# Folding the last query tile of an attention item by halves of its keys, in a kernel that runs attention beside two feed-forward layers

## The reference

```python
scores = scale * np.matmul(q, k.transpose(0, 1, 3, 2))
mask = (pos[:, None] // 64) >= (pos[None, :] // 64)
scores = np.where(mask, scores, -1000000000.0)
scores = scores - np.max(scores, axis=-1, keepdims=True)
attn = np.exp(scores)
attn = attn / (np.sum(attn, axis=-1, keepdims=True) + 1e-09)
x = np.matmul(attn, v)                      # to [2304 tokens, 512]
h = x @ moe_w_in                            # 512 x 2048
g = np.where(h >= 1, h, np.where(h <= -1, 0.0, (h + 1) ** 2 / 4.0))
x = g @ moe_w_out                           # 2048 x 512
h = x @ moe2_w_in
out = (h * np.cos(h)) @ moe2_w_out
```

## Time and profile before

| | |
|---|---|
| median of three runs | 1042.07 us |
| profiled execution, its own time | 1043.83 us |
| span of that execution, first to last instruction | 1041.7 us |
| PE busy | 997.8 us, 96% of the span |
| DVE busy | 657.9 us, 63% |
| ACT busy | 590.0 us, 57% |
| POOL busy | 422.7 us, 41% |
| mean granted TensorE clock | 0.988 of full |

### The profile page before, as it was taken

How to read it: one execution, slowest core, us unless ns; L and a number is a source line. 1 busy time by engine, 2 the same in 40 slices (tenths; PEclk the granted TensorE clock), 3 DMA queues, 4 the chain that set the end, 5 groups by cost and what they waited for, 6 DMA issues and landing times.

```text
span 1041.7 us, 19484 instructions
## 1 busy us (share of the span) xinstructions
PE 997.8 (96%) x7360; PEld 941.2 (90%) x7360; DVE 657.9 (63%) x1422; ACT 590.0 (57%) x1232; POOL 422.7 (41%) x446
## 2 busy tenths in 40 slices
PE   5699999999999999999999999999999999999997
PEld 4588999899999999999999999899999999999995
DVE  5668777766766767667642369665565656656553
ACT  5578766666666666666642357545445454545542
POOL 4558755655555554654632222222221222222221
PEclk9889999999999999999999999999999999999999
DMA  5235321221211212211110045010110101001000
GB/s 166 92 109 171 98 76 59 70 73 49 89 53 49 93 49 67 75 58 64 69 48 22 21 157 187 1 41 0 40 24 16 40 0 40 12 29 40 0 21 21
DMA packets 30885, 62.27 MB, mean 60 GB/s; under 512 B 3680, under 2 KB 11872, under 8 KB 30816
## 3 DMA queue, kind: packets, MB, share of 16 engines
q1 hardware_dynamic: 29664, 57.16, 17.2%
q10 hardware_dynamic: 1152, 4.19, 1.1%
HBM read 51.90 MB, written 9.44 MB: 59 GB/s over the span
## 4 chain that ended last, share of the span: by engine, by line
PE 79%; DVE 9%; ACT 5%; issue 3%; DMA 1%; POOL 1%; ACTq 0%; POOLq 0%; DVEq 0%
PE hidden L1155 33%; PE acc L1174 18%; PE acc L1188 13%; PE heads_out L1078 4%; PE scores L1032 3%; PE turned L1046 3%; PE scores L1033 2%; DVE neg_max L827 1%; PE heads_out L1046 1%; DVE wout_lo L892 1%; ACT probs L643 1%; DVE q_parts L816 1%; DVE x_lo L906 1%; PE hidden L1122 1%; DVE win_lo L885 1%
## 5 line engine op out<-in xcount | busy, mean ns | idle before, releaser
L568 POOL TENSOR_TENSOR g_lo<-work,g_hi 128x512 fp32r<-128x512 f32 x144 | 186.9, 1298 | 431.5 <-ACT g_hi L740 431.5
L1155 PE MATMUL hidden<-x_hi,win_hi 128*128 128x256 f32 x1136 | 321.9, 283 | 1.1 <-DVE work L917 1.1
L1155 PE MATMUL hidden<-x_hi,win_lo 128*128 128x256 f32 x1136 | 316.8, 279 | 3.8 <-DVE q_parts L816 2.8
L1155 PE MATMUL hidden<-x_lo,win_hi 128*128 128x256 f32 x1136 | 316.3, 278 | 0.0
L1155 PEld LDWEIGHTS hidden<-x_hi,win_hi 128*128 128x128 f32 x1136 | 214.6, 189 | 5.3 <-DVE work L917 1.3
L1155 PEld LDWEIGHTS hidden<-x_hi,win_lo 128*128 128x128 f32 x1136 | 214.6, 189 | 4.6 <-DVE q_parts L816 3.3
L1155 PEld LDWEIGHTS hidden<-x_lo,win_hi 128*128 128x128 f32 x1136 | 214.9, 189 | 3.8
L1188 PE MATMUL acc<-g_hi,wout_hi 128*128 128x256 f32 x576 | 167.5, 291 | 0.2 <-ACT y_stage L723 0.2
L1188 PE MATMUL acc<-g_hi,wout_lo 128*128 128x256 f32 x576 | 161.3, 280 | 3.0 <-DVE pt_lo L844 3.0
L538 POOL TENSOR_SCALAR probs<-probs,row_inv 64x576 f32<-64x576 f32 (+2 forms) x160 | 105.1, 661 | 136.8 <-DVE row_inv L839 135.9
L1188 PE MATMUL acc<-g_lo,wout_hi 128*128 128x256 f32 x576 | 160.5, 279 | 0.0
(11 more groups left out here) (99 smaller groups left out, 1841.2 us busy)
## 6 DMA issues: line engine op xcount, KB each, us to landing
qk_raw<-qk_late SPq DMA_DIRECT2D x32, 448.0 KB, 3.3
qk_raw<-qk_early SPq DMA_DIRECT2D x32, 256.0 KB, 2.6
v_raw<-v_late SPq DMA_DIRECT2D x32, 160.0 KB, 3.3
x_raw<-x_scratch SPq DMA_DIRECT2D x9, 512.0 KB, 3.4
out<-y_stage SPq DMA_DIRECT2D x36, 128.0 KB, 2.4
x_raw<-w_in SPq DMA_DIRECT2D x8, 512.0 KB, 3.6
y_stage<-w_out SPq DMA_DIRECT2D x8, 512.0 KB, 3.5
x_scratch<-y_stage ACTq DMA_DIRECT2D x8, 512.0 KB, 2.7
```

Of the source, the lines that this page charges most:

```text
L568: nc.gpsimd.tensor_tensor(g_lo[:, m % G_RING, :], work[:, m % 2, :], g_hi[:, m % G_RING, :], ALU.subtract).then_inc(g_lo_made, 1)
L1155: last = nc.tensor.matmul(into, w[:, p, c, half * P:(half + 1) * P], x[:, c, :], start=(i == 0), stop=(i == len(products) - 1))
```

## The change

Three parts, and a table of orders that goes with them.

**The fold.** Tile 4 of a late item becomes 128 rows by 320 keys. The keys are laid out in DRAM in the order of chunks 4, 0, 2, 1, 3. Rows 0 to 63 hold the 64 queries against chunks 4, 0 and 2, and rows 64 to 127 the same queries against nothing (the first 64 columns, masked), 1 and 3. PE gets this by two products into the same bank, with the queries shifted by 64 columns among zeros (`q_folded`): 320 columns and then 256. The row maxima and the row sums of the two halves are exchanged by copies of one column between the halves of the partitions (`max_swap`, `sum_swap`). Three transposes of 128 by 128 turn it, where five of 64 rows did. The queries of a late item are 384 columns where they were 320, with zeros among them. The score banks of late items alternate, so the first tile's scores no longer wait for the last exponential of the item before.

**Two buffers.** `k_hi`, `k_lo`, `qk_raw` and `v_raw` hold two late items. The raw data of the first two late items are loaded together after the split of item 31, and after that two items ahead. Keys of a late item are split at slots -14 and -13, before at -10 and -11.

**The last tile.** Pair 7 is made right behind pair 6, into a bank of `scores`; the last pair's 12 matmuls finish one accumulator bank and then the other, and each bank is copied and stored by itself.

```diff
-QKV_COLS = (2 * EARLY, LATE + S)
+LATE_Q = LATE + BLOCK
+QKV_COLS = (2 * EARLY, LATE_Q + S)
...
+KEY_ORDER = (4, 0, 2, 1, 3)
+KEY_COLS = [slice(P * j, min(S, P * (j + 1))) for j in KEY_ORDER]
+FOLD = LATE
...
-    return min(S, P * (i + 1))
+    return FOLD if i == 4 else P * (i + 1)
...
+def chunk_col(i, j):
+    return (0, 2 * P, P, 3 * P)[j] if i > 1 else P * j
...
-    "turn_c": (0, 0, 19), "weigh": (12, 18, 21), "k_hi": (-5, -9, -10), "q_hi": (-5, -8, -11),
...
-    "pt_lo_b": (0, 0, 18), "pt_lo_c": (0, 0, 19), "add": (13, 18, 23), "k_lo": (-4, -10, -11),
...
-    "begin": (16, -2, -6), "v_lo": (7, 7, 6),
...
+    "turn_c": (0, 0, 19), "weigh": (12, 17, 21), "k_hi": (-6, -9, -14), "q_hi": (-4, -8, -11),
...
+    "pt_lo_b": (0, 0, 18), "pt_lo_c": (0, 0, 19), "add": (13, 18, 23), "k_lo": (-4, -10, -13),
...
+    "begin": (16, -3, -10), "v_lo": (8, 8, 7),
...
+def keys_before(n):
+    return n - 3 if n < ALONE else -1 if n == ALONE else n - 2
...
-    if n + 1 < ITEMS:
-        yield n + 1, k - slots_of(n)
+    for m in range(n + 1, min(n + 3, ITEMS)):
+        yield m, k - sum(slots_of(i) for i in range(n, m))
...
-def slots_made(heads):
-    return {made_at(s, heads): s for s in range(PAIRS)}
+def slots_made(heads, last=False):
+    made = {made_at(s, heads): s for s in range(PAIRS)}
+    if last:
+        made[made_at(PAIRS - LAG - 2, heads) + 2] = made.pop(made_at(PAIRS - LAG - 1, heads))
+    return made
...
+        qk_raw = sb("qk_raw", [P, 2 * QKV_COLS[1]], F32)
+        v_raw = sb("v_raw", [P, 2 * 5 * D], F32)
+        q_parts = sb("q_parts", [P, 3, BLOCK + LATE_Q], F32R)
+        k_hi = sb("k_hi", [P, 2, S], F32R)
+        k_lo = sb("k_lo", [P, 2, S], F32R)
...
+        def hidden_of(m, last=False):
+            return scores[:, 0, :] if last and m == PAIRS - 1 else hidden[:, m % 2, :]
...
+        def q_tile(n, e):
+            at = 2 * BLOCK + BLOCK + P * e if late(n) else BLOCK + P * e
+            return q_parts[:, n % 3, at:at + P]
...
+        def q_folded(n, half):
+            at = BLOCK * (1 - half)
+            return q_parts[:, n % 3, at:at + P]
...
-            return (k_hi, g_hi[:, 0, EARLY:2 * EARLY], g_hi[:, 1, EARLY:2 * EARLY])[place_of(n)]
+            return (k_hi[:, n % 2 if n >= ALONE else 0, :], g_hi[:, 0, EARLY:2 * EARLY], g_hi[:, 1, EARLY:2 * EARLY])[place_of(n)]
...
+            return scores[:, (i + n) % 2 if late(n) else i % 2, 0:ext_of(i)]
...
+        def probs_fold(n, a):
+            at = probs_at(n, 4) + (BLOCK, BLOCK + P, 0)[a]
+            return probs[:, at:at + P]
...
+            def same_kind_of_raw(n):
+                return n < ITEMS and n not in (HEADS, HEADS + 1)
...
             def after_split(n):
                 sp.wait_ge(q_lo_made, n + 1)
                 sp.wait_ge(k_lo_made, n + 1)
-                if n + 2 < HEADS:
+                if same_kind_of_raw(n + 2):
                     load_qk(n + 2)
-                elif HEADS - 1 <= n < ITEMS - 1:
-                    load_qk(n + 1)
+                if n == HEADS - 1:
+                    load_qk(HEADS)
+                    load_qk(HEADS + 1)
...
             def store_out(t):
-                sp.wait_ge(acc_read, t + 2)
                 staged = y_stage[:, :].rearrange("p (a m) -> p a m", a=2)
                 for e in range(TOK // D):
+                    if e == 0 or (e == 2 and t == 2 * TILES - 1):
+                        sp.wait_ge(acc_read, t + 2 + e // 2)
                     row = out_rows(t - TILES, e)
                     sp.dma_start(out[row:row + D, :], staged[(e % 2) * D:(e % 2) * D + D, e // 2, :]).then_inc(y_stored, 16)
...
-                if user_before(n) >= 0:
-                    act.wait_ge(scores_made, first_tile(user_before(n) + 1))
+                if keys_before(n) >= 0:
+                    act.wait_ge(scores_made, first_tile(keys_before(n) + 1))
...
             def row_max(n, i):
                 tile = first_tile(n) + i - tiles_of(n)[0]
                 dve.wait_ge(scores_made, first_tile(n) + 2 if n < ALONE else tile + 1)
+                bank = bank_of(n, i)
+                if i == 4:
+                    hidden_part = bank[BLOCK:P, 0:BLOCK]
+                else:
+                    at = chunk_col(i, i) + BLOCK
+                    hidden_part = bank[0:BLOCK, at:at + BLOCK]
+                nc.vector.memset(hidden_part, MASKED).then_inc(masked, 1)
+                dve.wait_ge(masked, tile + 1)
+                col = stat(n, i)
+                top = neg_max[:, col:col + 1]
                 if i < 4:
...
+                    nc.vector.tensor_reduce(out=top, in_=bank, axis=AX_X, op=ALU.max, negate=True).then_inc(max_made, 1)
+                    return
+                m = n - HEADS + 1
+                nc.vector.tensor_reduce(out=top, in_=bank, axis=AX_X, op=ALU.max, negate=True).then_inc(half_max_made, 1)
+                dve.wait_ge(half_max_made, m)
+                for to, source in ((0, BLOCK), (BLOCK, 0)):
+                    nc.vector.tensor_copy(max_swap[to:to + BLOCK, :],
+                                          neg_max[source:source + BLOCK, col:col + 1]).then_inc(max_swapped, 1)
+                dve.wait_ge(max_swapped, 2 * m)
+                nc.vector.tensor_tensor(top, top, max_swap[:, :], ALU.min).then_inc(max_made, 1)
+            def inverse(n, i):
+                done = first_tile(n) + i - tiles_of(n)[0] + 1
                 dve.wait_ge(exp_made, done)
                 col = stat(n, i)
...
+                sums, inverses = row_sum[:, col:col + 1], row_inv[:, col:col + 1]
+                if i < 4:
+                    nc.vector.tensor_scalar_add(sums, sums, EPS).then_inc(sum_guarded, 1)
+                else:
+                    for to, source in ((0, BLOCK), (BLOCK, 0)):
+                        nc.vector.tensor_copy(sum_swap[to:to + BLOCK, :],
+                                              row_sum[source:source + BLOCK, col:col + 1]).then_inc(sum_swapped, 1)
+                    dve.wait_ge(sum_swapped, 2 * (n - HEADS + 1))
+                    nc.vector.scalar_tensor_tensor(out=sums, in0=sums, scalar=EPS, in1=sum_swap[:, :], op0=ALU.add,
+                                                   op1=ALU.add).then_inc(sum_guarded, 1)
                 dve.wait_ge(sum_guarded, done)
...
+                nc.vector.reciprocal(inverses, sums).then_inc(inv_made, 1)
...
+            def read_last(t, a, stored):
+                dve.wait_ge(acc_half_made, a + 1)
+                if a == 0:
+                    dve.wait_ge(y_stored, stored)
+                nc.vector.tensor_copy(y_stage[:, a * 512:(a + 1) * 512], acc[:, a, :]).then_inc(acc_read, 1)
...
-                        pe.wait_ge(exp_made, first_tile(n))
+                        pe.wait_ge(exp_made, first_tile(n) - (1 if n > ALONE else 0))
+                elif e == 1 and n > ALONE and not banks_seen(n):
+                    pe.wait_ge(exp_made, first_tile(n))
                 elif e == 2:
-                    pe.wait_ge(exp_made, first_tile(n) + 2)
+                    pe.wait_ge(exp_made, first_tile(n) + 1)
                 if i == 4:
...
+                    even, odd = q_folded(n, 0), q_folded(n, 1)
+                    width = S - FOLD
+                    products = [(bank, even, k[:, 0:FOLD]) for k in (k_hi_of(n), k_lo_of(n))]
+                    products += [(bank[:, FOLD - width:FOLD], odd, k[:, FOLD:S]) for k in (k_hi_of(n), k_lo_of(n))]
                 else:
...
+                    first = BLOCK if late(n) else 0
+                    products = [(bank, q_tile(n, e), k[:, first:first + ext_of(i)]) for k in (k_hi_of(n), k_lo_of(n))]
+                for which, (into, q, k) in enumerate(products):
+                    last = nc.tensor.matmul(into, q, k, start=(which == 0), stop=(which == len(products) - 1))
                 last.then_inc(scores_made, 1)
...
             def turn(n, e):
                 pe.wait_ge(probs_made, first_tile(n) + e + len(tiles))
...
+                if e == 2:
+                    sources = [probs_fold(n, a) for a in range(3)]
+                elif late(n):
+                    sources = [probs_chunk(n, tiles[0], j) for j in range(tiles[0] + 1)]
+                else:
+                    sources = [probs_chunk(n, i, j) for i, j in ((0, 0), (1, 0), (1, 1))]
+                for at, source in enumerate(sources):
+                    last = nc.tensor.transpose(turned_of(n, e)[:, at * P:(at + 1) * P], source, ident[:, :])
                 last.then_inc(turned_made, 1)
...
+            def use_last(t):
+                p, slot = PAIRS - 1, (PAIRS - 1) % G_RING
+                pe.wait_ge(g_lo_made, PAIRS * t + p + 1 + 2)
+                for a in range(TOK // P):
+                    for half in range(2):
+                        at = half * TOK + a * P
+                        for i, (w, g) in enumerate(((wout_hi, g_hi), (wout_hi, g_lo), (wout_lo, g_hi))):
+                            last = nc.tensor.matmul(acc[:, a, :], g[:, slot, at:at + P], w[:, p, half, :], start=False,
```

(19 more changed lines are left out.)

152 lines of the change are left out of this document (60 added, 92 removed).

## The result

The changed kernel takes 1074.84 us in the median of four runs (1074.04 to 1079.51) against 1042.43 us for the kernel before (1041.71 to 1043.18): a ratio of 1.032, 95% interval 1.0289 to 1.0351. It is 32 us slower; 12 us faster had been forecast.

The account below looks back on a forecast made before the run. PE's issue of matmuls was taken to bound the kernel. Fold -9.6, buffers -1.1, handover +1.1 and last tile -2.2 summed to -11.8 us, from the median of 1042.07 to 1030.3 us; range 1025 to 1037 us.

Parts of the forecast that it names:

- The fold on the other engines, at nothing: Late items: DVE gets about 0.65 us more per item, hidden beside PE's matmuls; ACT and POOL get less; cost nothing.
- The fold on PE: Tile 4 of late items: three transposes for five save 0.30 us in each of 32 items, 9.6 us.
- the rival by columns: Tile 4's transposes are paid by columns, so nothing is saved there; kernel lands at 1041.2 us; chance 6%.
- The four scores, cost "at nothing": Tile 4's four score products have 1152 columns in all before and after, so no change in time.
- Two buffers: Late items: PE's waits for the keys' low part go, as their split comes sooner; -1.1 us, ends -3.3 and 0.
- The handover: Start of late items: the wait for item 32's load is paid earlier, at a weighing; +1.1 us, ends 0 and +3.
- The last tile: End of program: less waiting for `g_lo` 1.0, shorter last copy 0.6, earlier stores 0.6; -2.2 us, ends -0.5 and -3.5.
- The table at 0 (±1.5): Early items' slots move by one or two on ACT, DVE and POOL; cost 0, with 1.5 us either side.
- The slower rival: New PE wait ahead of tile 4's transposes, low keys delaying POOL's normalising; at 0.6 us per item 1049.5 us; chance 8%.
- released by POOL: Sign that the forecast is wrong: PE idle ahead of tile 4's transposes, released by POOL, in many items.
- over 80%: Sign that the forecast is wrong: DVE busy for over 80% in the late stretch.

Follow-up runs that it names:

- no_swap: one_port_832 without the exchange of the two halves' maxima and sums, so the reference isn't computed for those 64 queries: 1029.90 us, ratio 0.9885.
- one_port_832: Changed kernel with the minimum and the sum taking the swapped column as a per-partition scalar, and 960 B of padding ahead of ident: 1041.32 us, ratio 0.9982.
- old_table: Changed kernel with the kernel before's table of slots put back: 1069.42 us, ratio 1.0262.
- tail_alone: Kernel before with only the last tile's part of the change: 1039.35 us, ratio 0.997.
- act_sums: one_port_832 with the two copies that exchange the halves' sums moved from DVE to ACT: 1052.94 us, ratio 1.0094.
- pad_64: Kernel before with 64 B of unused padding ahead of ident, no instruction changed: 1061.00 us, ratio 1.0177.
- all_64: Kernel before with 64 B of padding ahead of the weights, so that everything moves together: 1042.38 us, ratio 0.9999.

## Why the prediction was wrong

**The sum that failed.** Forecast 1030.3 us; measured in steps: place 16.2, the minimum behind POOL 17.3, the exchange 11.4 us. With them the forecast becomes 1075.2 us, and 1074.8 was measured. Without all three stands no_swap at 1029.9. That both agree within 0.4 us is partly luck: the terms that are left were off by up to some 2 us each and the table by 5.6 us, as shown below, and no_swap leaves out a step that the forecast had in it.

**"The fold on the other engines, at nothing"** is the step that failed worst, and in two places: priced at nothing, it cost 17.3 and 11.4 us. The minimum was priced at 147 ns from the row of an operation on one column. That row has one input; the minimum has two, and the table puts `k_lo` beside it. The trace of before had the pair of rows that shows it: of two instructions of one form in the second layer, both beside POOL's `g_lo` in 70 of 72 cases, the one with an input in PSUM takes 688 ns, and the one with both in SBUF takes 1166.

```profile
L929 DVE SCALAR_TENSOR_TENSOR work<-probs,work 128x512 f32<-128x512 f32 x72 | 84.0, 1166 | 2.5
...
L926 DVE SCALAR_TENSOR_TENSOR work<-probs,hidden 128x512 f32<-128x512 f32 x72 | 49.5, 688 | 7.5
```

The second place is the argument that 0.65 us per item "hides beside PE's matmuls" since DVE had 22 us idle in 75. The lengths were right: a copy takes 148 ns, the reduction 491, and DVE's load rose from 52.5 to 57 us (56.89 in one_port_832). But the idle time of an engine that works in order is no cover for what it does ahead of the instruction that PE waits for. The stretch already had five waits for `pt_lo`, so in some items there was no slack: some 1.1 us more ahead of `pt_lo` cost 11.4 / 32 = 0.36 us per item.

**The pace of a matmul was taken as fixed** is the other step that failed. No step of the prediction asked what the larger tensors do to those behind them, and no view of the trace of before shows it. This was 16.2 us. The range, 1025 to 1037, could not hold it. What in the memory makes the pace depend on the distance stays open.

**The fold on PE** was right in kind and too small. Around three transposes of 128 by 128 stand 0.37 us (0.36 forecast), so 0.29 us are saved (the medians of the late stretch are 0.66 and 0.37) and the rival by columns is out:

```profile
309.42 0.28 PE L1237 MATMUL hidden<-x_hi,win_lo 128*128 128x256 f32 x1
309.54 0.49 PE L1129 MATMUL turned<-ident,probs 128*128 128x128 f32 x3
309.79 0.36 PE L1270 MATMUL acc<-g_hi,wout_hi 128*128 128x256 f32 x1
```

One reading behind it was off. The 0.09 and 0.08 us "between two" transposes are whole groups divided by their count. A single one is busy for 0.22 us (64 columns) or 0.27 us, so by the earlier trace rows the last of the five starts at 305.44 and the last of the three at 301.71: the starts are 0.075 and 0.11 us apart. Columns do count inside a group. What the five lose is at their ends, 0.21 us ahead and 0.15 us behind, against 0.12 and 0.03.

The four scores, cost "at nothing" by their equal columns, take 0.53 us in every item of the changed kernel and 0.52 in one_port_832. The four of 288 columns took 0.53 us in 13 of 32 items and 0.63 to 0.64 in 19, where the second product starts 0.24 us behind the first instead of 0.13; the mean is 0.593 us. That is another 0.06 to 0.07 us, or some 2 us in 32 items. Why the second product was late in those 19 no run shows.

**Two buffers**: -1.1 us forecast for the waits for `k_lo`; they are gone. The two kernels with the old table have them again, 3.0 us in old_table.

**The handover**: +1.1 us forecast. From the copy of `acc` ahead of it to the one behind it, the kernel before takes 67.43 us, one_port_832 69.10 and no_swap 67.47: 0 to +1.7. The wait moved where it was forecast, with the load of item 32 issued 2.0 us later than before (178.60, not 176.59) and landing 5.0 us after that:

```profile
183.59 0.68 ACT L670 ACTIVATE k_hi<-qk_raw 128x576 fp32r<-128x576 f32 x1 [4.96 <-DMA qk_raw<-qk_late]
...
185.06 0.39 PE L1237 MATMUL hidden<-x_hi,win_lo 128*128 128x256 f32 x1 [2.54 <-POOL v_parts L594]
```

**The last tile**: -2.2 us forecast, -3.3 measured by tail_alone (1.9 to 4.5 by its interval), inside its ends. The wait for `g_lo` gave 0.5 us, not 1.0, and the way from the last matmul's start to the end 1.8 (6.3 to 4.4 us), not 1.2.

**The table at 0 (±1.5)** was mis-sized: -5.6 us with a fast minimum, +5.4 us with the slow one. These runs carry all of its entries, of the late items too, and not only the early ones that the prediction weighed.

**The slower rival** named the right place, the products ahead of tile 4's transposes, and the wrong path to it. It let POOL's `k_lo` delay POOL's own normalising; `k_lo` delayed DVE instead. Of its two signs, PE idle "released by POOL" and DVE "over 80%", neither showed: PE was released by DVE, at 77%.

## What to carry to other kernels

Ask of each added instruction not whether its engine has idle time but what stands behind it in that engine's queue and who waits for that; the busy share fell in act_sums and the kernel became slower. Before a small two-input instruction on DVE is priced, look at whether both inputs lie in SBUF and what POOL does at that moment; a per-partition scalar operand does the same work without waiting. When tensors change size, keep the distance between streamed operands and weights as it was, or measure a few pads: 64 B were worth 18.6 us of 1042, more than the change itself. Of the kernels here that compute the whole reference, the fastest is the kernel before with the last tile's part alone, 1039.35 us.

## What the runs showed of the hardware that was not expected

- The spacing of 128x256 matmuls hangs on the distance between the streamed operand and the weights in SBUF: 0.1144 us at 704 B modulo 1,024 and 0.1178 to 0.1197 us at 736, 768, 832 and 896 (second layer). The Trainium skill (SBUF — State Buffer, Who interferes with whom) has TensorE's reads wait for nobody and names the port shared by DVE and POOL as the only contention. The first is not borne out here as a rule of constant pace, since pad_64 differs from the kernel before in nothing but addresses; whether the two reads of TensorE meet in one part of the memory is a guess that fits all_64 and that no run proves.
- A DVE minimum of one column with two inputs in SBUF took up to 1.36 us beside a POOL instruction of 1.42 us, and 214 ns with one of them as a scalar per partition.
- Five transposes of 64 rows cost PE 0.66 us from the product ahead to the product behind and three of 128 rows 0.37 us, though the five start 0.075 us apart and the three 0.11: the difference lies ahead of the first and behind the last.
